# Mixer: router weights folded into the output projection, and a spatial product on full tiles of 128 rows

## What is computed

```python
h = np.maximum(x @ w_in, 0.0)
u, v = (h[..., :512], h[..., 512:])
v_n = (v - mean(v)) / np.sqrt(var(v) + 1e-06)
v_s = np.einsum('ts,bsd->btd', w_spatial, v_n) + b_spatial[None, :, None]
y = (u * v_s) @ w_out
logits = np.einsum('bsd,de->bse', y, w_gate)              # 8 columns
local_gate = sigmoid(y @ w_local)                         # 1 column
# token s takes argmax(logits) if s == 0 or local_gate < 0.5, else the expert of token s - 1
out = softmax(logits)[e] * (np.maximum(y @ w1[e], 0.0) @ w2[e])
```

## Time and profile before

| | |
|---|---|
| median of 3 runs | 1269.45 us (1269.32 to 1272.0) |
| profiled execution | 1270.8 us, span of its trace 1269.1 us |
| PE busy over the span | 1172.0 us, 92% |
| DVE, ACT, POOL busy | 785.4, 567.6, 537.0 us |
| mixer and routing, in the trace | about 592 to 951.5 us of the span |
| experts | from 951.5 us on |

### The profile page before, as it was taken

One profiled execution on the slowest core, in us unless ns is written; L12 is line 12 of the kernel. 1 busy time (PEld: TensorE's weight loads), 2 busy tenths in 40 slices (PEclk: granted clock), 3 DMA queues, 4 the chain that ended last, 5 costly groups with the idle time before them and its releaser, 6 DMA issues. The chain is left out here.

```text
span 1269.1 us, 23908 instructions
## 1 busy us (share of the span) xinstructions
PE 1172.0 (92%) x7459; PEld 1053.0 (83%) x7460; DVE 785.4 (62%) x1501; ACT 567.6 (45%) x1022; POOL 537.0 (42%) x597
## 2 busy tenths in 40 slices
PE   6999999999999999997889999999825999799997
PEld 5999999999999999996777989889714778577786
DVE  4888988888888888986532643526134532453532
ACT  4666666666666666663412223222105411341411
POOL 6777777777777777753100010100111520350400
PEclk9999999999999999998899999999856999899999
DMA  5121221212121221101301020120137531350110
GB/s 193 40 65 56 65 65 46 65 56 65 37 65 56 65 65 48 45 9 52 118 1 38 1 75 0 37 83 0 37 104 282 173 108 50 114 203 33 42 33 30
DMA packets 49579, 86.40 MB, mean 68 GB/s; under 512 B 8142, under 2 KB 20558, under 8 KB 49552
## 3 DMA queue, kind: packets, MB, share of 16 engines
q1 hardware_dynamic: 39264, 52.49, 13.2%
q0 software_dynamic: 5984, 19.95, 4.7%
q10 hardware_dynamic: 4304, 13.64, 3.0%
HBM read 69.77 MB, written 17.33 MB: 69 GB/s over the span
## 5 line engine op out<-in xcount | busy, mean ns | idle before, releaser
L618 DVE TENSOR_SCALAR_CACHE_REDUCE probs<-scores 128x1152 f32<-128x1152 f32 x144 | 195.5, 1358 | 61.0 <-PE scores L472 60.0
L472 PE MATMUL scores<-k_t,q_t 128*128 128x384 f32 x960 | 201.7, 347 | 1.3 <-DVE probs L618 1.3
L570 ACT ACTIVATE probs<-probs,neg_max 128x1152 f32<-128x1152 f32 x144 | 181.8, 1263 | 0.0
L594 ACT CAST pt_h<-ring 128x384 fp32r<-128x384 f32 x288 | 139.0, 483 | 73.6 <-PE ring L479 67.8
L495 PE MATMUL acc<-pt_h,v_parts 128*128 128x256 f32 (+1 forms) x576 | 169.3, 316 | 0.6 <-DVE pt_l L684 0.6
L479 PE MATMUL ring<-consts,probs 128*128 128x128 f32 x1296 | 165.4, 273 | 0.7 <-DVE pt_l L684 0.7
L472 PEld LDWEIGHTS scores<-k_t,q_t 128*128 128x128 f32 x960 | 160.7, 189 | 2.2 <-DVE probs L618 2.1
L495 PE MATMUL acc<-pt_l,v_parts 128*128 128x256 f32 (+1 forms) x576 | 157.2, 295 | 0.0
L328 POOL TENSOR_TENSOR pt_l<-mid,pt_h 128x384 fp32r<-128x384 f32 x144 | 145.5, 1010 | 12.0
L479 PEld LDWEIGHTS ring<-consts,probs 128*128 128x128 f32 x1296 | 146.2, 141 | 2.5 <-DVE pt_l L684 1.8
L684 DVE TENSOR_TENSOR pt_l<-ring,pt_h 128x384 fp32r<-128x384 f32 x288 | 145.8, 548 | 0.0
(11 more groups left out here) (195 smaller groups left out, 2530.3 us busy)
## 6 DMA issues: line engine op xcount, KB each, us to landing
w_raw<-moe_w POOLq DMA_DIRECT2D x10, 1024.0 KB, 6.2
k_nat<-k SPq DMA_DIRECT2D x32, 288.0 KB, 2.8
v_nat<-v SPq DMA_DIRECT2D x32, 288.0 KB, 2.8
q_nat<-q SPq DMA_DIRECT2D x32, 256.0 KB, 2.9
w_raw<-moe_w ACTq DMA_DIRECT2D x3, 2048.0 KB, 11.0
rows_in<-sorted_tokens SPq DMA_DIRECT2D x23, 257.0 KB, 2.6
x_in<-x_heads SPq DMA_DIRECT2D x18, 256.0 KB, 3.3
x_heads<-x_pair SPq DMA_DIRECT2D x16, 256.0 KB, 2.4
```

Of the source, the lines that this page charges most:

```text
L472: mm = nc.tensor.matmul(scores[:, c, 0:CK], q_t[par][:, side, t * P:(t + 1) * P], k_t[par][:, c * CK:(c + 1) * CK], start=(i == 0), stop=( ...
L570: nc.scalar.activation(probs[n % 3][:], probs[n % 3][:], ACT.Exp, bias=neg_max[:, n % 3:n % 3 + 1], scale=-1.0, accum_out=row_sum[:, n:n + ...
L594: nc.scalar.copy(pt_h[:, 3 * c:3 * c + 3, n * P:(n + 1) * P], ring[c][:, 0:CK].rearrange("p (i r) -> p i r", i=3)).then_inc(s["high_done"], 1)
L618: nc.vector.tensor_scalar(probs[n % 3][:], scores[:, :, 0:CK], -0.5 * DH ** -0.5, None, ALU.mult, ALU.min, accum_out=neg_max[:, n % 3:n % ...
```

## The change

Before the loop, `router_weights` transposes w_out on PE (16 transposes into four banks, ACT copies them into `wout_t`, which lies in the space of `y`), multiplies it by the router weights (16 float32 products of 12 columns: eight logits, the local gate, three zeros; 32 instructions on PE), and ACT and DVE split the result into 12 further columns of `wout_h` and `wout_l`. A y tile then has 524 columns, computed as two halves of 262 in two banks, with the same weights loaded for both; the logits are columns 512 to 520 of `y`. `turn_y`, `logit`, DVE's `project`, `y_t` and the tensor `logits` are gone. ACT copies a y tile in two pieces. The gate product of row group 0 moves behind the projection. `choose` waits for the last y copy.

The last projection interleaves the first two y tiles by k, with a wait for each k's gate tile.

`spatial` uses all 128 rows of the fifth tile; the rows from 64 on of `wsp_h` and `wsp_l` are zeroed once by DVE.

`placed` makes one product a tile, of nine columns (the place by expert, and their sum); `tag` finds the expert by comparing with zero. For that the sorted list starts at row 1. `placed` and `tag` move ahead of `first_x`, its low parts and the last m of `spatial`; `rank` computes `place` ahead of `carry`.

```diff
+YW = DM + E + 4
+YA = YW // 2
...
-    put("region", p * CAP - 1)
+    put("region", p * CAP)
+    put("pick", (p == np.arange(E + 1)[None]) | (np.arange(E + 1)[None] == E))
...
-    wout_h = sb("wout_h", [P, KD, DM], F32R)
+    wout_h = sb("wout_h", [P, KD, YW], F32R)
...
+    y = sb("y", [P, QT, YW])
+    logits = y[:, :, DM:DM + E + 1]
+    wout_t = y[:].rearrange("p t c -> p (t c)")[:, 0:KD * DM].rearrange("p (k n) -> p k n", k=KD)
...
+    router_out = tall[0][:, 0:KD * 16].rearrange("p (m c) -> p m c", m=KD)[:, :, 0:E + 4]
...
         def _(pe):
                     halves(wide[m % 2], [
-                        ((val_h[0:rows_of(t), t, cols], val_l[0:rows_of(t), t, cols]),
-                         (wsp_h[0:rows_of(t), t], wsp_l[0:rows_of(t), t]))
+                        ((val_h[:, t, cols], val_l[:, t, cols]), (wsp_h[:, t], wsp_l[:, t]))
                         for t in range(QT)]).then_inc(s["sp_done"], 1)
...
+            def y_part(t, ks):
+                cols = slice(t * P, (t + 1) * P)
+                for k in ks:
+                    for i, (g, w) in enumerate(((gate_h, wout_h), (gate_h, wout_l), (gate_l, wout_h))):
+                        for bank, part in ((tall, slice(0, YA)), (small, slice(YA, YW))):
+                            mm = nc.tensor.matmul(bank[t % 2][:, 0:YA], g[:, k, cols], w[:, k, part],
+                                                  start=(k == 0 and i == 0), stop=(k == KD - 1 and i == 2))
+                return mm
+
+            def project(b):
+                pe.wait_ge(s["gate_lo"], KD * (b + 1))
+                pe.wait_ge(s["v_relu"], QT * (b + 2))
+                for t in range(QT):
+                    if t >= 2:
+                        pe.wait_ge(s["y_ready"], QT * b + t - 1 + 1)
+                    y_part(t, range(KD)).then_inc(s["y_done"], 1)
+
+            def project_last(b):
+                pe.wait_ge(s["x_lo"], QT * B + 2)
+                pe.wait_ge(s["y_tagged"], 3 * b + 1)
+                for k in range(KD):
+                    pe.wait_ge(s["gate_lo"], KD * b + k + 1)
+                    for t in range(2):
+                        mm = y_part(t, (k,))
...
+            def router_weights():
+                for k in range(KD):
+                    bank = (tall + small)[k]
+                    for m in range(KD):
+                        mm = nc.tensor.transpose(bank[:, m * P:(m + 1) * P], wout_raw[:, m, k * P:(k + 1) * P], ident)
+                    mm.then_inc(s["wout_turned"], 1)
+                pe.wait_ge(s["wout_t_ready"], KD)
+                pe.wait_ge(s["small_loaded"], 48)
+                for m in range(KD):
                     for k in range(KD):
+                        mm = nc.tensor.matmul(tall[0][:, m * 16:m * 16 + E + 4], wout_t[:, k, m * P:(m + 1) * P],
+                                              wgate[:, k], start=(k == 0), stop=(k == KD - 1))
+                mm.then_inc(s["wlogit_done"], 1)
...
             def placed(b):
-                    nc.tensor.matmul(small[0][:, 16 * t:16 * t + E], onehot[:, cols],
-                                     ident[0:E, 0:E], start=True, stop=True)
-                    mm = nc.tensor.matmul(small[0][:, 16 * t + E:16 * t + E + 1], place[:, cols],
-                                          const("ones", E)[:, 0:1], start=True, stop=True)
+                    mm = nc.tensor.matmul(small[0][:, 16 * t:16 * t + E + 1], place[:, t * P:(t + 1) * P],
+                                          const("pick", E), start=True, stop=True)
...
             pe.wait_ge(s["win_lo"], 2)
             pe.wait_ge(s["wsp_lo"], QT)
+            pe.wait_ge(s["wout_loaded"], 16)
+            router_weights()
+            pe.wait_ge(s["wlogit_hi"], 2)
+            pe.wait_ge(s["wout_lo"], 1)
             gates(0, 0)
             spatial(0)
...
             with pe.Fori(0, B - 1) as b:
                 values(b + 1)
-                project(b, False)
-                gates(b + 1, 1)
+                project(b)
+                gates(b + 1, 0)
                 spread(b)
                 spatial(b + 1, range(KD - 1))
+                placed(b)
                 first_x(b + 2)
                 spatial(b + 1, range(KD - 1, KD))
-                placed(b)
-            project(B - 1, True)
+            project_last(B - 1)
...
         def _(act):
-                    nc.scalar.copy(y[:, t, 0:DM], tall[t % 2][:]).then_inc(s["y_ready"], 1)
+                    nc.scalar.copy(y[:, t, 0:YA], tall[t % 2][:, 0:YA])
+                    nc.scalar.copy(y[:, t, YA:YW], small[t % 2][:, 0:YA]).then_inc(s["y_ready"], 1)
...
+            nc.scalar.copy(wout_h[:, :, 0:DM], wout_raw).then_inc(s["wout_hi"], 1)
+            for k in range(KD):
+                act.wait_ge(s["wout_turned"], k + 1)
+                nc.scalar.copy(wout_t[:, k], (tall + small)[k][:]).then_inc(s["wout_t_ready"], 1)
+            act.wait_ge(s["wlogit_done"], 1)
+            nc.scalar.copy(wout_h[:, :, DM:YW], router_out).then_inc(s["wlogit_hi"], 1)
             normalise(0)
...
         def _(dve):
+            for buf in (wsp_h, wsp_l):
+                nc.vector.memset(buf[REM:P, QT - 1].bitcast(F32), 0.0).then_inc(s["zeroed"], 1)
...
+            dve.wait_ge(s["wlogit_hi"], 1)
+            nc.vector.tensor_tensor(wout_l[:, :, DM:YW], router_out, wout_h[:, :, DM:YW].bitcast(F32), ALU.subtract
+                                    ).then_inc(s["wlogit_hi"], 1)
             normalise(0)
...
                 values(b + 1)
-                project(b)
                 choose(b)
                 normalise(b + 1)
                 rank(b, b + 2)
                 spatial(b + 1, range(KD - 1))
+                tag(b)
                 for t in range(2):
                     x_low(b + 2, t)
                 spatial(b + 1, range(KD - 1, KD))
-                tag(b)
```

More of the change, by code:

```diff
@@ L64 @@
     ("place", E + 2),
+    ("pick", E + 1),
 ):
@@ L802, in write_padding @@
             at = e + PADDING * LIST
-            row = eng.value_load(counts[0:1, at:at + 1], min_val=0, max_val=E * CAP - P)
+            row = eng.value_load(counts[0:1, at:at + 1], min_val=0, max_val=E * CAP + 1 - P)
             eng.dma_start(sorted_dram[bass.ds(row, P)], pad_row[:]).then_inc(s["padded"], 16)
@@ L952, in spatial @@
                     halves(wide[m % 2], [
-                        ((val_h[0:rows_of(t), t, cols], val_l[0:rows_of(t), t, cols]),
-                         (wsp_h[0:rows_of(t), t], wsp_l[0:rows_of(t), t]))
+                        ((val_h[:, t, cols], val_l[:, t, cols]), (wsp_h[:, t], wsp_l[:, t]))
                         for t in range(QT)]).then_inc(s["sp_done"], 1)
[L957 to L964, removed]
-                        pe.wait_ge(s["y_ready"], QT * b + t - 1 + 1)
[L966 to L974, removed]
-                    for k in range(KD):
[L976 to L1004, removed]
@@ new lines, in project @@
+            def project(b):
[3 more added lines that the diff above has]
+                    if t >= 2:
+                        pe.wait_ge(s["y_ready"], QT * b + t - 1 + 1)
+                    y_part(t, range(KD)).then_inc(s["y_done"], 1)
[6 more added lines that the diff above has]
+                        mm = y_part(t, (k,))
+                        if k == KD - 1:
+                            mm.then_inc(s["y_done"], 1)
+                for t in range(2, QT):
+                    pe.wait_ge(s["y_ready"], QT * b + t - 1 + 1)
+                    y_part(t, range(KD)).then_inc(s["y_done"], 1)
@@ L1230, in spatial @@
                                             ALU.subtract).then_inc(s["gate_lo"], 1)
-            def project(b):
-                def take_logits(t):
-                    dve.wait_ge(s["l_done"], QT * b + t + 1)
-                    nc.vector.tensor_copy(logits[:, t], small[1][:, 0:E + 1]).then_inc(s["logits_ready"], 1)
-                for t in range(QT):
-                    dve.wait_ge(s["y_turned"], QT * b + t + 1)
-                    if t >= 1:
-                        take_logits(t - 1)
-                    nc.vector.tensor_copy(y_t[:].rearrange("p k r -> p (k r)"), small[0][:]
-                                          ).then_inc(s["y_t_ready"], 1)
-                take_logits(QT - 1)
             def choose(b):
@@ L1293, in rank @@
                 then(nc.vector.tensor_tensor_scan(chain, keeps, codes, 0.0, ALU.mult, ALU.add))
-                then(nc.vector.tensor_scalar(onehot[:, 0:T], chain, const("expert1", E), None, ALU.is_equal))
-                then(nc.vector.tensor_tensor_scan(ranks, onehot[:, 0:T], onehot[:, 0:T], carry[:],
-                                                  ALU.add, ALU.max))
+                then(nc.vector.tensor_scalar(onehot[:], chain, const("expert1", E), None, ALU.is_equal))
+                then(nc.vector.tensor_tensor_scan(ranks, onehot[:], onehot[:], carry[:], ALU.add, ALU.max))
+                then(nc.vector.scalar_tensor_tensor(
+                    out=place[:, 0:T], in0=ranks, scalar=const("region", E), in1=onehot[:],
```

(6 more changed lines are left out.)

40 lines of the change are left out of this document (17 added, 23 removed).

## The result

The changed kernel takes 1224.9 us, median of four runs (1224.35 to 1225.79); the kernel before, beside it on the same chip, takes 1269.38 (1268.95 to 1272.0). The ratio is 0.9652, 95% interval 0.9634 to 0.967: faster by 3.5%. The profiled execution is 1225.79 us for a span of 1223.7, so the span fell by 45.4 where the terms gave 38.0.

A forecast was written before the change was run, and what follows sets the result against it. PE was taken to set the time inside the loop. Terms 8.2 - 2.7 - 28.0 - 13.3 - 2.2 = -38.0 took the profiled 1270.8 us to 1232.8, a predicted median of 1231.5; range 1222 to 1241.

The forecast's parts named there:

- a sign that I had named as wrong: Signs against the forecast included a full clock where it was kept slow; no size given for the sign.
- the clock comes back: Rival: light stretch keeps the clock, three passes gain 1.7 us each, router products up to 5.3; 1226.4 to 1221; chance 0.2.
- Projection in the loop: Loop projection: five tiles of 24 matmuls at 0.122 us, then the gate product, 17.9 us for 23.67; -5.8 a pass.
- The dear rival: Rival: a matmul's price does not shrink with its columns, 262 costing 0.234 us; +54, 1285 us; chance 0.03.
- Full tiles: Spatial product: without changes of rows, 0.38 us a half product, each of four batches saves 2.7 us.
- `placed`, -1.2: `placed` in the loop: ten of 20 instructions remain, 1.16 us for 2.32; -1.2 us a pass.
- New wait: Before a pass's spatial product: late exponentials delay the value split, so PE waits about 0.35 us; +0.35 a pass.
- The clock in the loop: Loop passes: the 2.0 us light stretch still loses the clock, now within the spatial product; loss left in place.
- Last projection: After S, end of the last spatial product: buffers free at S+6.5, choosing at S+17.2 instead of 30.5 us; -13.3.
- Tail: After the last projection: `placed` loses ten of 20 small matmuls at half clock, 0.22 us each; -2.2 us.
- Before the loop: Router work delays gates, one stop and clock loss go, first spatial product at 651.1; +8.2 us, bounds -5.3 and +2.
- Experts: Experts after the tail: not edited, so predicted change 0.

The follow-up runs named there:

- the projection's part alone: Kernel after with the fifth spatial tile on 64 rows and `placed` in 20 instructions at its old place: 1250.07 us, ratio 0.984.
- the 12 columns: Kernel after with the projection's 524 columns cut as 512 and 12 instead of 262 and 262: 1249.07 us, ratio 0.9838.
- forwards and backwards: Fifth spatial tile on all 128 rows in the kernel before: 1258.22 us; back on 64 rows in the kernel after: 1236.29 us.
- late `placed`: Kernel after with the ten `placed` matmuls, and `tag`, back behind the last spatial product of each pass: 1230.03 us, ratio 0.9684.
- full tiles alone: Kernel before with only the fifth spatial tile on all 128 rows, padding rows zeroed once: 1258.22 us, ratio 0.9888.
- the router's work was hidden: Kernel after with w_out transposes between turned wsp tiles and router products behind the first spatial product: 1222.26 us, ratio 0.9617.
- `placed` twice: Kernel after with each product of `placed` made twice, 20 instructions for 10, at its new place: 1233.2 us, ratio 0.9692.
- short `placed`: Kernel before with only `placed` cut from 20 instructions to 10, at its old place: 1263.06 us, ratio 0.9931.
- once more: Kernel after, unchanged, run again as base for the next three runs: 1226.56 us, ratio 0.9656.

## Why the prediction was right, and where its sizes were off

The forecast's mechanism held: PE bounds the loop, and each matmul taken out of its queue came off the end. 1231.5 was 6.6 us above the median of the runs. 1224.9 lies inside the range but 3 below the forecast's own (1228 to 1235), and a sign that I had named as wrong did show, a full clock where I kept it slow: half of the difference is the rival *the clock comes back*. By its steps:

- **Projection in the loop, -5.8.** Measured -5.8 from the first matmul of the projection to the first of `spread` (833.47 to 866.91 before, 813.97 to 841.63 after, all gates in it), and -5.3 with that part alone, which has the new wait too. 0.122 for 262 columns, from the rows at 256 and 288, was right. The dear rival (0.234 for any width) is out; what is true in it is a floor near 0.11, which the 12 columns show.
- **Full tiles, -2.7 a batch.** -2.9, shown twice, forwards and backwards. The narrow matmuls save nothing, and each change of rows costs 0.08 to 0.10 us beyond a step at the first matmul behind it and 0.10 to 0.11 at the next.
- **`placed`, -1.2.** -1.1 in place. **New wait, +0.35.** 0.57, some 0.5 more than before, and the experiment that moves the exponentials shows that they cause it, as the prediction said.
- **The clock in the loop, 0.** Here the term was mis-sized: "I leave the loss in place". The light stretch of 2.06 us never lost the clock. In the second and third pass, whose falls before stand at 740.9 and 816.0, that gives 1.5 each, 3.1 in all; these passes fell by 10.9, and 9.4 of it is work, where I had 9.3. The first pass fell by 10.0 (75.18 to 65.20). It starts at half clock in both kernels behind PE's wait for x, 3.4 us of it before and 2.9 after, so that only 0.3 of it is clock. The three passes gave 3.7 more than the term, and 3.4 of that is clock. The sum also had a slip here: the third fall of before lies outside the three passes, while a loss kept in place would have lain within all of them, so "in place" would have cost about 1.5 more than 0. The rival's 1.7 for each of three passes is thus right as a price of keeping the loss, and too much as a correction of the sum. I had put 2.0 us "nearer to 2.32" than to the 1.2 behind which the clock held; in the runs it held behind 2.0 us in all passes, and fell behind 2.3 and more in most.
- **Last projection, -13.3.** -13.7: with S at 861.59, buffers free at S+6.3 (S+6.5), the stall 0.91 instead of 1.5, no clock loss. The late `placed` shows that the early tag is worth 6.1 us there, less 1.3 by which it lengthens the stretch before S (3.5 of the whole time). With the projection's part alone it is 25.0 us from the last spatial matmul to the first of `spread`, against 34.9 before: 9.9 by the shorter tile list and the interleaving, with 3.4 us of half clock in it instead of 6.8; no run separates these.
- **Tail, -2.2.** -2.1: ten instructions in 2.30 at half clock.
- **Before the loop, +8.2.** +4.6, or +6.0 with the 1.4 of the stage before, in which the half clock reached 3.3 us into values(0) instead of 0.9. The router products took 4.56 instead of 7.0, since the clock was full at their start (0.80 over all of them), inside the bounds that I gave but not where I stood. That the clock loss behind the stop for ACT would go was wrong: the half clock moved ahead of the gates and became longer. The longer half clock at the start of values(0) is there with full tiles alone on the kernel before too, and is absent where the router's work was hidden, so I do not lay it on the change.
- **Experts, 0.** -0.9; its cause stays open.

The sum of the differences is -7.4: -3.7 in the three passes, nearly all of it clock, -2.2 before the first spatial product, -0.9 in the experts, and small ones. From 589 us to the end of the last projection's tiles the low-clock stretches add up to 41.0 us before and 30.7 after, which at half the length bounds the clock's part of the 45.4 us at about 5; the rest is work and waits taken out.

What stays open is why the clock falls behind the same list of matmuls in one pass and not in the next (two of three with full tiles alone, two of three with `placed` twice). Each rests on one trace; the runs give how often, not what decides it.

## What to carry to other kernels

Where PE is busy for 99% of a loop, price an edit by the steps between starts at the same shape, and look for starts that step wider than their neighbours: the changes from 128 to 64 rows and back cost 0.37 us a half product, and the narrow matmuls saved nothing. Cut an awkward width evenly (262 and 262, not 512 and 12): here 12 columns cost half of what 512 did. Count the small matmuls between two wide stretches as a price of their own. Before you leave a clock loss in the sum, run the kernel with a shorter and a longer stretch of them, and note in which stage each fall lies.

## What the runs showed of the hardware that was not expected

- Stretches of small matmuls and transposes in the loop, by length: 1.2 us, the clock held in all four where a wide stretch followed at once (short `placed` and late `placed`), and fell in the third pass of both, where PE then stood idle for 1.9 and 2.3 us; 2.0 us, it held in all 21 (the kernel after, once more, and five of its variants); 2.3 to 3.4 us, it fell in 10 of 12, in seven of them with PE never idle. A fall put PE at 1.2 GHz for 3.4 us, at the cost of 1.5 to 1.6, or for 6.8.
- 12 columns with a weight load of their own cost 0.11 us behind a matmul of 512, nearly what 256 columns take (0.119).
- fp32 products of 12 columns: 4.24 us for 32 where the clock was full until the last third, and 4.56 at a mean clock of 0.80; at half clock throughout, small ones take 0.22 to 0.23 each (ten in 2.30).
- A slow clock can hide a wait: with `placed` late, PE at half clock reached the buffer 0.57 us too early, where in the projection's part alone, at half clock for half as long (3.4 us), it waited 1.96.
